# First two slot tiles listed from five token tiles, and routing moved into tile 0's first product, in an attention, expert and mixing kernel

## What is computed

```python
# 1. attention, 8 heads of 64: window of +-15 keys plus 24 block summaries
a = softmax(concat(scale * q @ k.T masked to |i-j| < 16, scale * q @ k_max_of_32 + log 32))
x = a @ concat(v, v_mean_of_32)
# 2. experts: each token takes one of 8 experts
for s in range(S):
    fresh_e = argmax(logits[b, s])
    e = fresh_e if s == 0 or local_gate[b, s] < 0.5 else prev_e
    prev_e = e
    out[b, s] = softmax(logits)[e] * (relu(x[b, s] @ w1[e]) @ w2[e])
# 3. mixing: theta = x @ w_theta; z = x * (cos, sin)(theta); token mixing with two
#    768x768 matrices; u = x + y; u + relu(u @ w_ch)
```

## Time and profile before

| | us |
|---|---|
| median of 3 runs (422.81 to 424.49) | 423.3 |
| the profiled execution | 423.85 |
| its span, first to last instruction | 422.1 |
| PE busy in it | 410.7 (97%) |
| DVE busy | 257.5 (61%) |
| ACT busy | 194.2 (46%) |
| POOL busy | 74.5 (18%) |

### The profile page before, as it was taken

The page is one execution under the profiler, slowest core; times in us unless marked ns, Lnnn a source line. Parts: engine busy times, 40 slices in busy tenths (PEclk is TensorE's granted clock), DMA queues, the critical chain, the costliest instruction groups (busy, mean ns, idle before and its releaser), DMA issues.

```text
span 422.1 us, 8098 instructions
## 1 busy us (share of the span) xinstructions
PE 410.7 (97%) x2791; PEld 329.0 (78%) x2792; DVE 257.5 (61%) x429; ACT 194.2 (46%) x431; POOL 74.5 (18%) x115
## 2 busy tenths in 40 slices
PE   7898999999999999999999999999999999999996
PEld 3677787468887888888888778888888888888885
DVE  4898997898646327363117595666687646454352
ACT  1698995624647326463247464444433143213110
POOL 2688950221112100121110022200000000000000
PEclk9999999999999999999999999999999999999999
DMA  8995552172989933518130025300000000000012
GB/s 289 392 396 176 176 185 76 52 248 77 382 277 403 374 132 98 200 39 334 50 100 26 0 66 196 113 2 0 0 2 0 26 25 0 27 25 27 25 58 93
DMA packets 18191, 54.50 MB, mean 129 GB/s; under 512 B 2032, under 2 KB 2160, under 8 KB 17904
## 3 DMA queue, kind: packets, MB, share of 16 engines
q1 hardware_dynamic: 14288, 44.13, 29.0%
q0 software_dynamic: 2000, 6.56, 5.2%
q10 hardware_dynamic: 1872, 3.41, 2.1%
HBM read 40.46 MB, written 13.63 MB: 128 GB/s over the span
## 4 chain that ended last, share of the span: by engine, by line
PE 87%; DVE 4%; ACT 4%; issue 2%; DMA 1%; DVEq 1%; POOL 0%; SPq 0%; ACTq 0%; POOLq 0%
PE ps L1573 15%; PE ps L1575 15%; PE ps L1574 15%; PE ps L1717 8%; PE ps L1719 8%; PE ps L1718 8%; PE ps L1435 3%; PE ps L1655 2%; PE ps L1595 2%; PE ps L1416 2%; PE ps L1406 2%; PE ps L1624 2%; PE ps L1463 2%; DMA kfull<-k_full 1%; ACT p L708 1%
## 5 line engine op out<-in xcount | busy, mean ns | idle before, releaser
L1717 PE MATMUL ps<-z_h,mix_h 128*128 128x512 f32 x144 | 56.9, 395 | 0.0
L1719 PE MATMUL ps<-z_h,mix_l 128*128 128x512 f32 x144 | 56.1, 390 | 0.0
L1718 PE MATMUL ps<-z_l,mix_h 128*128 128x512 f32 x144 | 56.1, 390 | 0.0
L1573 PE MATMUL ps<-w_h,hT_h 128*128 128x512 f32 x104 | 42.0, 404 | 0.9 <-DVE w_l L1098 0.8
L1098 DVE TENSOR_TENSOR w_l<-w_raw,w_h (+1 forms) x32 | 37.4, 1219 | 8.4 <-ACT w_h L759 8.4
L708 ACT ACTIVATE p<-s,nmax 128x120 f32<-128x120 f32 x96 | 36.5, 385 | 11.5 <-DVE nmax L941 11.5
L1575 PE MATMUL ps<-w_l,hT_h 128*128 128x512 f32 x104 | 40.7, 391 | 0.0
L1574 PE MATMUL ps<-w_h,hT_l 128*128 128x512 f32 x104 | 40.5, 390 | 0.0
L1573 PE MATMUL ps<-w_h,xT_h 128*128 128x512 f32 x96 | 38.4, 400 | 0.0
L1574 PE MATMUL ps<-w_h,xT_l 128*128 128x512 f32 x96 | 37.4, 390 | 0.0
L1575 PE MATMUL ps<-w_l,xT_h 128*128 128x512 f32 x96 | 37.4, 390 | 0.0
(11 more groups left out here) (263 smaller groups left out, 855.3 us busy)
## 6 DMA issues: line engine op xcount, KB each, us to landing
w_raw<-w SPq DMA_DIRECT2D x32, 512.0 KB, 5.7
mix_raw<-mix SPq DMA_DIRECT2D x6, 768.0 KB, 5.7
kfull<-k_full SPq DMA_DIRECT2D x8, 400.0 KB, 6.6
q_all<-q_t SPq DMA_DIRECT2D x6, 512.0 KB, 7.5
vpad<-v_pad SPq DMA_DIRECT2D x4, 768.0 KB, 8.9
xd<-x_sb SPq DMA_DIRECT2D x12, 256.0 KB, 2.5
ys<-y_sb ACTq DMA_DIRECT2D x12, 256.0 KB
out<-o SPq DMA_DIRECT2D x12, 256.0 KB, 2.0
```

The lines of the kernel that those rows point to most:

```text
L1573: pe.matmul(ps[:, bank, :], a_h[:, k, :], w_h[:, n, :], start=(k == 0), stop=False)
L1717: pe.matmul(ps[:, i, :], w_h, zh, start=(jb == 0 and m == 0), stop=False)
L1718: pe.matmul(ps[:, i, :], w_h, zl, start=False, stop=False)
L1719: mm = pe.matmul(ps[:, i, :], w_l, zh, start=False, stop=(jb == TPB - 1 and m == 1))
```

## The change

- The first slot list is made from FROM = 5 token tiles instead of six, and every step of it runs one tile of the attention earlier: on DVE the copy of the logits, the maxima and the fresh flags in tile 7, the keys at the end of tile 8, the scan in tile 9, the choice in tile 10, ranks, lanes and the final copy in tile 11; on the PE `first_turn` in tile 9, `first_back` in tile 10, `first_rank` and `first_list` in tile 11.
- In tiles 10 and 11 two copies of transposes change their place or engine.
- Of the six `keep_warm` matmuls between the attention and tile 0's product one stays. `routing_turn`, `routing_back` and `routing_ranks` stand between the matmuls of that product.
- `w1_step(0)` runs on DVE before the last logits copy, `w1_step(1)` and `w1_step(2)` in the two waits of the routing, `xT_copy(1)` inside the slot arithmetic, `w1_step(3)` after it. `routing_list` stands in the middle of `product1(1)`, `transpose_slots(2)` in the middle of `product2(0)`, and on DVE `xT_copy(2)` one instruction earlier.
- The weights of slot tile 2 are chosen by one comparison (`N_THIRD`, semaphore `third_ready`), and the wait on `table_ready` stands behind `product2(1)`.
- One more small matmul counts expert 0 in the first five tiles.

```diff
+FROM = TPB - 1
-WARM, WARM_SUM, WARM_SLOTS = (5, 1), (1, 0), (3, 1, 1, 1)
+WARM, WARM_SUM, WARM_SLOTS = (5, 1), (1, 0), 1
...
# POOL
+                if g == NT - 1:
+                    pool.wait_ge(x0_saved, 16 * TPB)
+                    pool.wait_ge(olist_done, 1)
+                    load_first(0)
...
# ACT
-                if 1 < g <= SUMMARY_TILES:
+                if 1 < g <= SUMMARY_TILES or g == NT - 1:
                     pT_copy(g, 1)
...
-            xaT_copy(NT - 1)
-            act.sem_inc(xTf_h, 1)
             act.wait_ge(scores_ready, NT)
             for i in range(STEPS):
+                if i == STEPS // 2:
+                    xaT_copy(NT - 1)
+                    act.sem_inc(xTf_h, 1)
...
# DVE, tile(g)
+                if g == NT - 2:
+                    pT_copy(g, 0)
+                    pT_copy(g, 1)
+                if g == NT - 1:
+                    first_ranks()
+                    first_lanes()
                 inverse(g, s)
...
-                if g == NT - 2:
+                if g == NT - 3:
                     first_scan()
-                if g == TPB + 2:
+                if g == FROM + 2:
                     first_logits(g - 2)
...
+                if g == NT - 2:
+                    first_choice()
                 if g == NT - 1:
-                    first_choice()
+                    first_list()
                 norm(g)
...
             lg_copy(NT - 2)
-            first_ranks()
-            first_lanes()
+            w1_step(0)
             lg_copy(NT - 1)
-            first_list()
...
-            w1_step(0)
+            w1_step(1)
             dve.wait_ge(vT_ready, 1)
...
+            w1_step(2)
             dve.wait_ge(back_ready, 1)
...
-            w1_step(1)
             dve.wait_ge(count_ready, 1)
...
+            dve.tensor_scalar(table[0:1, N_TILES, N_THIRD:N_THIRD + 1], r_end[0:1, 0, 0:1], float(FIRST_TILES * P), None, ALU.is_le)\
+               .then_inc(third_ready, 1)
             dve.scalar_tensor_tensor(r_base[:, :], r_end[:, 0, :], -1.0, r_al[:, 0, :], ALU.add, ALU.subtract)
             link(dve.tensor_tensor(r_rest[:, :], r_end[:, 0, E - 1:E], r_end[:, 1, E - 1:E], ALU.subtract))
+            xT_copy(1)
...
-            w1_step(2)
-            xT_copy(1)
+            w1_step(3)
             dve.wait_ge(list_ready, 1)
...
-            w1_step(3)
             hT_copy(0)
...
# PE, tile(g)
+                if g == NT - 1:
+                    first_rank()
                 transpose_p(g, s, first)
+                if g == NT - 2:
+                    first_back()
...
-                if g == NT - 2:
+                if g == NT - 3:
                     first_turn()
                 if g == NT - 1:
-                    first_back()
+                    first_list()
                 weigh(g, first)
...
-            keep_warm(WARM_SLOTS[0])
-            routing_turn()
-            keep_warm(WARM_SLOTS[1])
-            routing_back()
-            keep_warm(WARM_SLOTS[2])
             transpose_slots(0, first=True)
-            keep_warm(WARM_SLOTS[3])
-            routing_ranks()
+            keep_warm(WARM_SLOTS)
...
+                    if (c, k) == (0, 0):
+                        routing_turn()
+                    if (c, k) == (0, 1):
+                        routing_back()
+                    if (c, k) == (1, 0):
+                        routing_ranks()
+                    if (c, k) == (1, 1):
                         transpose_slots(1)
...
-            routing_list()
-            product1(1, 0)
-            transpose_slots(2)
-            product2(0, 0, first=True)
+            product1(1, 0, middle=routing_list)
+            product2(0, 0, first=True, middle=lambda: transpose_slots(2), at=KF // 2)
             transpose_h(1)
-            pe.wait_ge(table_ready, 1)
-            product1(2, place_of(2))
+            pe.wait_ge(third_ready, 1)
+            product1(2, pe.value_load(table[0:1, N_TILES, N_THIRD:N_THIRD + 1], min_val=0, max_val=1))
             transpose_slots(3)
             product2(1, 0)
+            pe.wait_ge(table_ready, 1)
```

More of the change, by code:

```diff
@@ L156, in program @@
         overlay = at[0]
[L157 to L174, removed]
+        o_lg = sb("o_lg", [P, FROM, E + 1])
+        o_m = sb("o_m", [P, FROM])
+        o_t = sb("o_t", [P, FROM])
+        o_u = sb("o_u", [P, FROM])
+        o_f = sb("o_f", [P, FROM])
+        o_v = sb("o_v", [P, FROM])
+        o_scan = sb("o_scan", [FROM, P])
+        o_carry = sb("o_carry", [P, FROM + 1])
+        o_w = sb("o_w", [P, FROM], i32)
+        o_e = sb("o_e", [P, FROM], i32)
+        o_oe = sb("o_oe", [P, FROM], bf16)
+        o_cum = sb("o_cum", [P, FROM], bf16)
+        o_off = sb("o_off", [P, FROM])
+        o_slot = sb("o_slot", [P, FROM], u32)
+        o_tile = sb("o_tile", [P, FROM], u32)
+        o_lane = sb("o_lane", [P, FROM], u32)
+        o_in = sb("o_in", [P, FROM, FIRST_TILES])
+        o_ot = sb("o_ot", [P, FROM, FIRST_TILES], fp16)
         at[0] = overlay
@@ L1065, in first_list, with split_step, w1_step @@
                 dve.tensor_copy(slot_list[:, 0:FIRST_TILES], ps[:, B_O, P + 24:P + 24 + FIRST_TILES]).then_inc(olist_done, 1)
+            def split_step(n, i, raw, hi, lo, hi_done, done):
+                dve.wait_ge(hi_done, n + 1)
+                dve.tensor_tensor(lo[:, bass.ds(i * SW, SW), :], raw[:, bass.ds(i * SW, SW), :],
+                                  hi[:, bass.ds(i * SW, SW), :].bitcast(f32), ALU.subtract).then_inc(done, 1)
+            def w1_step(i):
+                split_step(i, i, w1_raw, w1_h, w1_l, w1_hi, w1_split)
             dve.memset(warm, 1.0).then_inc(warm_done, 1)
@@ L1205, in _ @@
                 split_step(i, i, w2_raw, w2_h, w2_l, w2_hi, w2_split)
+            xT_copy(2)
             dve.tensor_tensor(r_ls[:, :, :], lge, m_b, ALU.subtract).then_inc(lse_ready, 1)
-            xT_copy(2)
             link(dve.scalar_tensor_tensor(r_end[0:1, 1, :], r_end[0:1, 1, :], r_rest[0:1, :], r_al[0:1, 1, :], ALU.add, ALU.subtract))
@@ L1478, in first_rank @@
                 pe.wait_ge(ocum_ready, 1)
-                pe.matmul(ps[:, B_O, P + 16:P + 16 + TPB], tri_b[:, :], o_oe[:, :], start=True, stop=False)
-                pe.matmul(ps[:, B_O, P + 16:P + 16 + TPB], ones_b[:, :], o_cum[:, :], start=False, stop=True).then_inc(orank_ready, 1)
+                pe.matmul(ps[:, B_O, P + 16:P + 16 + FROM], tri_b[:, :], o_oe[:, :], start=True, stop=False)
+                pe.matmul(ps[:, B_O, P + 16:P + 16 + FROM], ones_b[:, :], o_cum[:, :], start=False, stop=True).then_inc(orank_ready, 1)
             def first_list():
                 pe.wait_ge(olanes_ready, 1)
-                for j in range(TPB):
-                    mm = pe.matmul(ps[:, B_O, P + 24:P + 24 + FIRST_TILES], o_ol[:, j, :], o_ot[:, j, :], start=(j == 0), stop=(j == TPB - 1))
+                for j in range(FROM):
+                    mm = pe.matmul(ps[:, B_O, P + 24:P + 24 + FIRST_TILES], o_ol[:, j, :], o_ot[:, j, :], start=(j == 0), stop=(j == FROM - 1))
                 mm.then_inc(olist_ready, 1)
@@ L1527, in _ @@
             route_logits(NT - 2)
-            first_rank()
             transpose_x(NT - 1)
@@ L1549, in routing_ranks @@
                 pe.matmul(ps[:, B_R, R_RANK:R_RANK + E * NT], ones_b[:, :], r_cum[:, :, :].rearrange("p e j -> p (e j)"), start=False, stop=True)
-                pe.matmul(ps[:, B_R, R_COUNT:R_COUNT + V], ones_b[:, :], r_cum[:, :, TPB - 1:NT:TPB], start=True, stop=True).then_inc(count_ready, 1)
+                pe.matmul(ps[:, B_R, R_COUNT:R_COUNT + V], ones_b[:, :], r_cum[:, :, TPB - 1:NT:TPB], start=True, stop=True)
+                pe.matmul(ps[:, B_R, R_COUNT + V:R_COUNT + V + 1], ones_b[:, :], r_cum[:, 0, FROM - 1:FROM], start=True, stop=True).then_inc(count_ready, 1)
             def routing_list():
@@ L1575, in product, with product1 @@
                 return pe.matmul(ps[:, bank, :], a_h[:, k, :], w_l[:, n, :], start=False, stop=(k == last))
-            def product1(t, place):
+            def product1(t, place, middle=None):
                 pe.wait_ge(xTf_taken, t + 1)
@@ L1580, in product1 @@
                 for k in range(KD):
+                    if middle and k == KD // 2:
+                        middle()
                     pe.wait_ge(w1_split, place * STEPS + (STEPS + k + 1))
@@ L1596, in transpose_h, with product2 @@
                 mm.then_inc(hT_ready, 1)
-            def product2(t, place, first=False, middle=None, bank=B_Y):
+            def product2(t, place, first=False, middle=None, at=KF // 4, bank=B_Y):
                 if not first and bank == B_Y:
@@ L1601, in product2 @@
                 for k in range(KF):
-                    if middle and k == KF // 4:
+                    if middle and k == at:
                         middle()
```

71 lines of the change are left out of this document (29 added, 42 removed).

## The result

| | before | after |
|---|---|---|
| median, 22 runs each on one chip | 423.38 us (422.36 to 425.4) | 425.0 us (422.93 to 425.88) |
| profiled execution | 423.85 us, span 422.1 | 423.75 us, span 421.8 |
| PE busy in the span | 410.7 us | 406.8 us |

The ratio is 1.0032, 95% interval 1.0022 to 1.0042: 1.6 us slower by the medians and 1.4 by the means, which is less than half a per cent. The forecast was 420.7, with a range from 419.3 to 422.9. It is missed, and on the other side.

What follows compares the result with a forecast made beforehand. The PE was taken as the bound, busy 410.7 of 422.1 us, partly with filler awaiting the first list. 4.1 earlier, less 0.6 routing, 0.25 + 0.55 waits and rounding, and 0.05, gives 2.6: 420.7 us, range 419.3 to 422.9.

Steps and rivals of the forecast that it cites:

- Parts 1 and 2: Attention's end to product 0: the list's copy runs 3.5 us earlier, at 69.95; product 0 starts at 76.25, 4.1 earlier.
- Part 3: Routing inside product 0: the PE never waits for DVE; the product ends at 84.25, 3.5 us earlier.
- Part 4: After product 0, DVE is late: PE waits of 0.25 and 0.55; `product2(0)` ends at 98.3, 2.65 us left.
- Part 5: Behind `product2(0)`: the next expert's load moves little, but slack of 2.75 just holds the 2.65 gained; 0.05 us lost.
- The load 0.25 earlier: SP's load of the next expert's weights is issued only 0.25 us earlier than 103.19.
- ACT has 1.7 to give, since the last quarter arrives near 111: Rounding the next expert's weights: last quarter arrives near 111, ACT needed it at 112.7, so 1.7 us of slack.
- Rival B: Next expert's weights late: last quarter at 112, not 111; tile 2's second product moves by 1.5 only; 421.8 us, chance 0.15.
- DVE has 0.8 of slack over ACT: DVE's copies for tile 2 have about 0.8 us more slack than ACT's.
- Rival D: With `keep_warm` matmuls removed the PE's clock falls, halved for product 0: +7.0, 427.7 us; chance 0.04.
- Rival E: Expert 0's tokens spill and one slot tile is added: about 12.3 us more, 433.0 us; chance 0.02.
- The sign named for a wrong middle: The prediction's middle is wrong if product 0 starts after 77.5 or the PE waits for DVE or ACT between 105 and 120.

Runs made afterwards that it cites:

- the filler: Three unused matmuls of 512 columns added ahead of tile 3's first product in the changed kernel; 424.83 us, ratio 1.0035.

## Why the prediction was wrong, step by step

- **Parts 1 and 2** held to a quarter of a microsecond: the list's copy at 69.69 (69.95 forecast), the gather's transposes at 74.59 (74.8), product 0 at 76.1 (76.25), the waits for logits and gather 0.41 and 0.20 (0.55 for the latter). The steps in between held too: weighting 9 came 0.21 later than before, weighting 10 at 65.55 and weighting 11 at 69.55 (0.2, 65.5 and 69.6 forecast).
- **Part 3** held: product 0 ends at 84.3 (84.25) and waits nowhere for DVE.
- **Part 4** held within 0.45: the wait ahead of the list 0.36 (0.25), `product2(0)` at 92.70 (92.3) after a wait of 0.44 (0.55), its end at 98.74 (98.3). Gained there: 2.05 of the forecast 2.65; 0.16 of the difference is that the forecast compared with the chain's 100.95 where the timeline has 100.79.
- **Part 5 failed**, the step that gave tile 2's copies enough slack to take up what the PE had gained. It had three terms that together were to hold 2.75 us. *The load 0.25 earlier*: it was 0.37 later. The transposes came at 95.53, as forecast (95.5), but I had left out ACT's copy of them, 0.6, ahead of DVE's. *ACT has 1.7 to give, since the last quarter arrives near 111*: it arrived at 112.67, later than rival B's 112 too. By the chain above, the issue of the fourth quarter begins at 105.12 (the first at 103.56), and 7.53 pass until it has landed. I had counted 5.5 and 2 from 103.5, 1.6 us too early. An estimate for the kernel before, with the same 9.11 from its issue at 103.19, puts the last quarter at 112.3, when ACT took it at 112.7: 0.4 to give and not 1.7. *DVE has 0.8 of slack over ACT*: there is none. The slack was read from when ACT and DVE worked on the weights, but what the PE waits for stands behind them: 3.7 us of register loads and 1.6 of `chosen()` on DVE, and the same loads on ACT, which showed in the trace of before as idle time put down to "issue" ahead of `hT_h` and `r_s`. I had not read those rows. In the kernel before, the first half of `hT_l` (119.26, 0.7 long) was ready at 119.96 and the product began at 120.08: the chain ended just ahead of the PE, so next to nothing of what the PE gained could pass it. The term for this step was 0.05; it is 2.2. Moving the loads and `chosen()` gave 2.2 back in the changed kernel and nothing that can be told in the kernel before.
- **Rival B** has half of the mechanism, with a price of 1.1: weights late behind a table that does not move. With weights as late as that but nothing behind them tile 2's product did not wait, so the other half, the loads and `chosen()`, was in none of the rivals.
- **Rival D** named the second loss, at the wrong place: I looked for an idle stretch where the filler matmuls had been, and priced it with product 0. There the longest gap is 0.41. The clock falls at the wait of 2.0 to 2.6 at tile 2, in 14 of the first 22 executions, and costs 1.5 to 2.2, not 7. No trace showed the Trainium skill's rule at work when it was cited ("TensorE: Matmul & The Clock Gate", Part 1: idle halves the clock, activity releases it); these runs do, with 0.50 behind a wait of 2.64 us and within one of 4.15, and the full clock again after some microseconds of matmuls.
- **Rival E** did not come (the PE has 2781 matmuls against 2791 before); its price was read from a stretch that is tile 1's second and tile 3's first product, not tile 2's two, which as one period of the loop is as long (12.3).
- The sign named for a wrong middle, a PE that waits for DVE between 105 and 120, is the one that came.

The sum as it should have been, for the profiled execution: 2.05 gained to `product2(0)`'s end, less 2.2 at tile 2, nothing left (423.75 against 423.85). The medians differ by 1.6. The clock has about 0.7 of it, from the 424.27 of the eight executions at full clock to the 425.0 of all; the other 0.9, by which those eight stand above the kernel before, is not accounted for.

## What to carry to other kernels

Follow a gain to the next place where another engine hands something to the PE, and ask there what starts that engine's chain. Idle time named "issue" in front of an instruction is work too (here register loads at about 0.75 us each), and it is slack only if its start moves with the rest. And before a wait is moved or made, look at what the matmul engine does meanwhile: in this kernel a wait of 2.0 to 2.6 us came with a spell at half clock in 25 of 46 executions, which one profile at the full clock doesn't show; read the clock of all runs.

## What was not expected of the hardware

- In three kernels whose profiled PE waits 2.0 to 2.6 us at tile 2, the mean clock was below 0.999 in 14 of 22, 4 of 12 and 7 of 12 executions, in one with a wait of 4.15 us in 6 of 6; in four with none over 0.81 us at this place in 0 of 38 (the three kernels with the register loads moved, and the filler), and in the kernel before in 2 of 48.
- The fall can come late: behind the wait of 2.64 the PE had worked at the full clock for 0.8 us again when it halved; at that of 4.15 it had halved during the wait.
- A load of a register from SBUF costs an engine about 0.75 us, here 0.6 to 0.9 (five in 3.7 us on DVE, two more 1.5 us on ACT).
- Holding back the second four of a load's eight DMAs (512 KB each) brought nothing for the first four: 9.1 us from the first issue to the last quarter with and without.
